# Attention and two expert layers on one core: GpSimd splits queries before values, and five pieces of operand work change their place

## What is computed

```python
# q, k, v: 4 x 8 x 576 x 64; block-causal mask, blocks of 64
scores = q @ k^T / sqrt(64); masked where block_i < block_j
x = softmax(scores) @ v                     # -> 2304 x 512
p = probs / (sum(probs) + 1e-9)
for e in range(4):
    y += p[:, e] * (relu(x @ w1[e]) @ w2[e])  # 512 -> 1024 -> 512
h = y @ w_in
ln = layer_norm(h * softmax(h)) * g_ln
out = ln @ w_out
```

## Time and profile before

| what | value |
|---|---|
| median of the runs | 1160.57 us |
| time of the profiled execution | 1159.74 us |
| its span, from first to last instruction | 1157.9 us |
| PE busy, share of the span | 1138.7 us, 98% |
| PE busy, first 185 us (attention) | 175.23 us |
| PE busy, 185 to 262 us | 73.24 us |
| PE busy, 262 to 935 us | 673.00 us |
| DVE / ACT / POOL busy, first 185 us | 165.25 / 158.05 / 163.12 us |

### The profile page before, as it was taken

One profiled execution on the slowest core, in us unless ns is written; L12 is line 12 of the kernel. 1 busy time (PEld: TensorE's weight loads), 2 busy tenths in 40 slices (PEclk: granted clock), 3 DMA queues, 4 the chain that ended last, 5 costly groups with the idle time before them and its releaser, 6 DMA issues.

```text
span 1157.9 us, 16760 instructions
## 1 busy us (share of the span) xinstructions
PE 1138.7 (98%) x6131; PEld 1020.9 (88%) x6131; DVE 633.4 (55%) x1139; ACT 428.5 (37%) x943; POOL 415.7 (36%) x403
## 2 busy tenths in 40 slices
PE   8999998989999999999999999999999999999998
PEld 7999988879999999999999999999998977888887
DVE  8999886454343424343433344353424468666765
ACT  7988885322223211122311113321112344434432
POOL 7998996654234100015300004500003463432330
PEclk9999999999999999999999999999999999999999
DMA  4766767983734222252405062503125100000001
GB/s 142 227 213 211 218 207 221 393 323 124 277 113 157 89 82 110 82 194 72 180 1 191 1 230 71 200 28 132 60 83 199 39 16 10 29 19 28 19 28 37
DMA packets 68342, 146.29 MB, mean 126 GB/s; under 512 B 6064, under 2 KB 34736, under 8 KB 68272
## 3 DMA queue, kind: packets, MB, share of 16 engines
q1 hardware_dynamic: 68272, 145.36, 36.2%
HBM read 114.60 MB, written 30.74 MB: 126 GB/s over the span
## 4 chain that ended last, share of the span: by engine, by line
PE 76%; POOL 1%; DVE 1%; DMA 1%; ACT 0%; issue 0%; SPq 0%; ACTq 0%; POOLq 0%
PE s L1723 34%; PE outp L1584 19%; PE s L1584 11%; PE ring L1584 10%; PE ring L1854 1%; DMA xr<-x_stash 1%; PE s L1797 1%; POOL x_late L761 0%; DMA x_stash<-x_tmp 0%; POOL yop_l L863 0%; DVE yop_l L1432 0%; ACT y_t L1108 0%; DVE acc L1378 0%; POOL x_tmp L785 0%; DVE ex L1504 0%
## 5 line engine op out<-in xcount | busy, mean ns | idle before, releaser
L1723 PE MATMUL s<-xr,w1s 128*128 128x384 f32 x2016 | 360.8, 337 | 4.9 <-DVE u L1414 2.5
L1723 PEld LDWEIGHTS s<-xr,w1s 128*128 128x128 f32 x2016 | 351.9, 189 | 9.7 <-DVE u L1414 2.8
L1061 ACT ACTIVATE hid_h<-u 128x384 fp32r<-128x384 f32 x96 | 50.4, 525 | 371.9 <-DVE u L1409 346.7
L720 POOL TENSOR_TENSOR work<-work 128x256 f32<-128x256 f32 x20 | 15.9, 797 | 393.8 <-DMA work<-in_moe_w 267.9
L1364 DVE SCALAR_TENSOR_TENSOR hid_l<-s,hid_h 128x384 fp32r<-128x384 f32 x48 | 26.7, 557 | 125.7 <-ACT hid_h L1057 125.7
L1723 PE MATMUL s<-w1s,yop_h 128*128 128x512 f32 x252 | 85.7, 399 | 1.9 <-POOL yop_l L863 0.7
L1322 DVE TENSOR_TENSOR u<-s,m_b 128x384 f32<-128x384 f32 x24 | 13.4, 557 | 131.9 <-PE s L1723 131.9
L1057 ACT ACTIVATE hid_h<-s 128x384 fp32r<-128x384 f32 x48 | 23.6, 491 | 155.6 <-PE s L1584 155.6
L1584 PE MATMUL s<-k_h,qb 128*128 128x288 f32 (+8 forms) x320 | 75.9, 324 | 3.3 <-ACT pr L906 1.7
L906 ACT ACTIVATE pr<-s,neg_max 128x576 f32<-128x576 f32 (+2 forms) x144 | 75.5, 537 | 3.3 <-DVE neg_max L1206 3.0
L1584 PE MATMUL outp<-w_h,hid_h 128*128 128x512 f32 x192 | 75.5, 393 | 0.0
(11 more groups left out here) (172 smaller groups left out, 2446.2 us busy)
## 6 DMA issues: line engine op xcount, KB each, us to landing
xr<-x_stash SPq DMA_DIRECT2D x77, 768.0 KB, 6.4
r_sb<-r_scratch SPq DMA_DIRECT2D x16, 576.0 KB, 4.3
x_rows<-x_n SPq DMA_DIRECT2D x32, 288.0 KB, 4.6
work<-x_rows SPq DMA_DIRECT2D x24, 384.0 KB, 6.7
x_stash<-x_tmp SPq DMA_DIRECT2D x12, 768.0 KB, 3.8
work<-in_moe_w SPq DMA_DIRECT2D x32, 256.0 KB, 3.9
stage<-in_moe_w SPq DMA_DIRECT2D x32, 256.0 KB, 5.1
x_stash<-xr SPq DMA_DIRECT2D x7, 768.0 KB, 9.8
```

What stands on the lines that cost most here:

```text
L720: pool.tensor_tensor(s1, a21, a22, ALU.add).then_inc(w1_sums, 1)
L1061: act.activation(hid[slot][0][:, :], source, ACT.Relu).then_inc(hid_high, 1)
L1723: last = pe.matmul(target, x, y, start=start and i == 0, stop=stop and i == 2, skip_group_check=True)
```

## The change

1. GpSimd's round p of the attention does `split_query(p + 2)` before `split_values(p)`. The query split no longer waits for `v_split`; at the start of a round GpSimd waits for its own last work of the round before.
2. SP issues `load_q(p + 3)` right behind `load_k(p + 2)`, before `store_r(p)`, and no longer behind `load_v(p + 1)`.
3. GpSimd's `x_low_part(0, 0, 2)` and `(0, 0, 3)` move from round 13 to round 12, before `x_join(0, 1)`. After the attention `x_join(sg + 1, 0)` moves behind `x_low_part(sg, 1, 2)` and `(sg, 1, 3)`.
4. ACT's `x_cast(0, 1, 0)` moves from the end of step 13 to its middle, `x_cast(0, 1, 3)` from the end of step 14 to `nearly_late` of it.
5. SP stores group 0's slots in the pieces 0 to 2, 3, 4, and 5 to 6, with rounds of group 1 between them, not in two pieces 0 to 2 and 3 to 6.
6. DVE's `normalise_probs` (seven small operations, L1355 to L1359) moves from unit 2 to unit 4, just before its first user.

```diff
--- before.py
+++ after.py
@@ -583,6 +583,8 @@
                     load_x(0, 1, (0,))
                 if p + 2 < PAIRS:
                     load_k(p + 2)
+                if p + 3 < PAIRS:
+                    load_q(p + 3)
                 store_r(p)
                 spread_r(p)
                 if p == 11:
@@ -593,8 +595,6 @@
                     store_x(p - 1)
                 if p + 1 < PAIRS:
                     load_v(p + 1)
-                if p + 3 < PAIRS:
-                    load_q(p + 3)
                 if p in (1, 3, 5):
                     v_ = (p + 1) // 2
                     if v_ >= 2:
@@ -622,12 +622,16 @@
             stash_round(1, 0, 1)
             sp.wait_ge(w2_ready, 4)
             load2(w2[0, :, :], 3)
-            stash_first(range(3, NP))
+            stash_first(range(3, 4))
             stash_round(1, 0, 2)
             stash_round(1, 0, 3)
             load_x(2, 0)
-            for r in range(NR):
-                stash_round(1, 1, r)
+            stash_first(range(4, 5))
+            stash_round(1, 1, 0)
+            stash_round(1, 1, 1)
+            stash_first(range(5, NP))
+            stash_round(1, 1, 2)
+            stash_round(1, 1, 3)
             load_operands(1)
             load_x(2, 1)
             for t in range(2):
@@ -687,7 +691,6 @@
                 pool.wait_ge(q_loaded[p % 2], 16 * (p // 2 + 1))
                 if p >= 2:
                     pool.wait_ge(scored, GROUPS_S * (p - 1))
-                    pool.wait_ge(v_split, p - 1)
                 else:
                     pool.wait_ge(crossed_clear, 1)
                 placed = [[heads_of(qb_l[p % 2] if z else qb_h[p % 2], 0, BLOCKS)[h * DH:(h + 1) * DH, :, h, :]
@@ -790,9 +793,21 @@
             pool.wait_ge(first_split, 3)
             split_query(1)
             for p in range(PAIRS):
-                split_values(p)
+                if p in (1, 3, 5, 7):
+                    pool.wait_ge(w1_ready, 3 * (p // 2) + 1)
+                if p in (2, 4, 6, 8):
+                    pool.wait_ge(w1_ready, 3 * (p // 2))
+                if p == 9:
+                    pool.wait_ge(v_split, 9)
+                if p in (10, 13):
+                    pool.wait_ge(x_added, 1 + p // 13)
+                if p == 11:
+                    pool.wait_ge(x_sums, 4)
+                if p == 12:
+                    pool.wait_ge(x_low, 2)
                 if p + 2 < PAIRS:
                     split_query(p + 2)
+                split_values(p)
                 if p in (0, 2, 4, 6):
                     w1_add(0, p // 2)
                     w1_low_first(0, p // 2)
@@ -808,10 +823,10 @@
                     x_low_part(0, 0, 0)
                     x_low_part(0, 0, 1)
                 if p == 12:
+                    x_low_part(0, 0, 2)
+                    x_low_part(0, 0, 3)
                     x_join(0, 1)
                 if p == 13:
-                    x_low_part(0, 0, 2)
-                    x_low_part(0, 0, 3)
                     x_add(0, 1, 0)
                     x_add(0, 1, 1)
                 if p == 14:
@@ -829,10 +844,10 @@
                     x_low_part(sg, t, 1)
                     if t == 0:
                         x_join(sg, 1)
-                    elif sg + 1 < SUPERS:
-                        x_join(sg + 1, 0)
                     x_low_part(sg, t, 2)
                     x_low_part(sg, t, 3)
+                    if t == 1 and sg + 1 < SUPERS:
+                        x_join(sg + 1, 0)
             def y_add(p):
                 t1, t2, t4 = (y_s[:, x * BLK:(x + 1) * BLK] for x in (0, 1, 3))
                 b21, b22 = y_t[:, BLK:2 * BLK], y_t[:, 3 * BLK:4 * BLK]
@@ -971,22 +986,21 @@
                     w1_cast_sums(0, p // 2)
                 if p in (10, 11):
                     x_cast(0, 0, p - 10)
-                if p == 14:
-                    x_cast(0, 1, 1)
+                if p in (13, 14):
+                    x_cast(0, 1, p - 13)
 
             def nearly_late(p):
                 if p == 11:
                     x_cast(0, 0, 2)
                 if p == 14:
                     x_cast(0, 1, 2)
+                    x_cast(0, 1, 3)
 
             def late(p):
                 if p in (0, 2, 4, 6):
                     w1_cast_plain(0, p // 2, 1)
                 if p == 11:
                     x_cast(0, 0, 3)
-                if p in (13, 14):
-                    x_cast(0, 1, 3 * (p - 13))
 
             def step(p, par, ahead=True):
                 n = p + 1
@@ -1398,9 +1412,9 @@
                         dve.wait_ge(x_low, NR * 2 * SUPERS)
                         for s in range(2):
                             dve.wait_ge(tmp_stored[s], 16 * 4 * (SUPERS - 1))
+                    if n == 1:
+                        normalise_probs()
                     accumulate(n - 1, 0, downs(m - 1, 2))
-                if m == 2:
-                    normalise_probs()
                 make_u3(m)
                 if m == 0:
                     scale_left(PAIRS - 1, 1)
```

## The result

The changed kernel takes 1155.19 us, median of 5 runs from 1152.29 to 1155.85, where the kernel before took 1160.54 beside it: a ratio of 0.9949, 95% interval 0.9935 to 0.9962. It is faster by 5.4 us, where 9.5 were forecast. The profiled execution took 1155.19 us, its span 1153.4 (before: 1157.9).

The account below looks back on a forecast made before the run. PE is busy 98% of the span, so only its waits and slow running could go: 5.3 us from stores and join plus 4.2 from the attention, 1160.57 - 9.5 = 1151.1 us; range for 8 in 10, 1148.0 to 1157.5.

Parts of the forecast that it names:

- What bounds the kernel: Whole kernel: PE is busy for 98% of the span, so only its waits and lower-clock time can be gained.
- Attention, 4.2 us: Attention, all pairs: queries first and moved x work gain 4.2 us, bounds 1 and 6.
- the lead at T8R of step 7: Attention, pairs 0 to 10: queries first put PE ahead by 0.7 us, bounds -1 and 1.5.
- Step 14: Attention, step 14: GpSimd's sums done earlier, ACT's and PE's waits go, all_right(14) comes sooner; 1.5 us.
- the last step: End of the attention: GpSimd's last low part ends earlier, PE's wait before its first `up` nearly goes; 1.3 us.
- The bounding argument that found 164.8: Attention, round 13: values end near 164.8 behind moved low parts and join, so PE is at most about 1.4 us ahead.
- The stall of unit 3, 4.19 us: Unit 3: with stores in pieces ACT's store lands earlier, so PE's wait and the slow stretch go; 4.19 us.
- The rival that the stall stays: Unit 3: the landing is late whatever stands behind, only the attention gains; 1156.4, chance 0.12.
- the one that the attention gains nothing: Attention: late values eat its gain, the gain from the stores stays; 1155.3, chance 0.05.
- normalise_probs, 0 us: Unit 4: normalise_probs before three `acc` operations is covered by DVE's spare time; 0 us, else some tenths lost.
- Unit 4, 1.07 us: Unit 4: earlier stores put the slots of m1, m6 and m2 in place before PE needs them; 1.07 us gained.
- a clock below 1 between 215 and 262 us: Units behind the attention: a granted clock below 1 at 215 to 262 us would show the forecast wrong.

Follow-up runs that it names:

- 3: Changed kernel with group 0's slots of m1, m6 and m2 stored first, the other four behind group 1's first three loads; 1157.34 us, ratio 0.9973.
- experiment 11: Kernel before with only queries split before values on GpSimd and load_q right behind load_k; 1155.83 us, ratio 0.9969.
- 1: Kernel before with only group 0's stores in pieces and x_join(2, 0) behind the low parts; 1158.04 us, ratio 0.9983.
- 6: Kernel of 1 with the x rows of group 2 loaded behind load_operands(1); 1157.51 us, ratio 0.9982.
- 9: Kernel before with stores in pieces, x_join(2, 0) behind the low parts and normalise_probs in unit 4, attention as before; 1156.95 us, ratio 0.9980.
- 4: Changed kernel with one more 768 KB copy out of xr, to a place nobody reads, behind group 0's last piece; 1156.66 us, ratio 0.9968.
- 5: Changed kernel with the load of group 2's x rows (1.57 MB) moved behind load_operands(1); 1152.04 us, ratio 0.9929.
- 7: Changed kernel with GpSimd splitting values before queries in rounds 7 and 13 alone; 1154.29 us, ratio 0.9947.
- 8: Kernel of 5 with GpSimd splitting values before queries in rounds 7 and 13; 1149.88 us, ratio 0.9918.
- 12: Kernel of 5 with GpSimd splitting values before queries in round 13 alone; 1150.36 us, ratio 0.9919.

## Why the prediction was half right

The time lies in the range (1148.0 to 1157.5) and on the faster side, but 0.7 us outside the forecast's own range, 1148 to 1154.5.

**What bounds the kernel: right.** PE's own work did not change; what moved is its waiting and its slow stretches.

**Attention, 4.2 us: right, 4.71, in part by luck.** Kernels with this attention code have m5 of unit 0 at 191.3 to 191.9, and once at 194.02 (3); those with the one before at 195.05 to 196.83. By steps: the lead at T8R of step 7 was 1.4 us (91.33 to 89.89) for 0.7 forecast, inside the bounds. At `all_right(13)` it was 2.0 for 1.4, with the values' end at 164.07 for 164.8, which did pace PE. Step 14 brought 0.8 of the 1.5 (182.68 - 171.11 = 11.57 us became 10.74), the last step 1.6 for 1.3: one term too small and one too large made the sum come out. The load of x rows no longer holds up the keys, and PE no longer waits for GpSimd before its first `up`. What the forecast did not weigh is the alternative: it took the whole block as one, and in experiment 11, without the moved low parts, the profile gains 6.2, 1.5 more. The bounding argument that found 164.8 had the term in it, 2.8 us in front of the values of pair 13.

**The stall of unit 3, 4.19 us: gone as forecast,** and ACT's store lands earlier: its cast starts at 221.04 for 230.41, 5.2 us earlier against PE, inside the 3 to 6 that the forecast named, and PE's way to m7 of unit 3 is 3.60 us shorter. The rival that the stall stays is wrong, though its time (1156.4) is near the result; so is the one that the attention gains nothing, whose 1155.3 is nearest of all.

**normalise_probs, 0 us: wrong as a term.** The seven operations took 2.7 us in unit 2 and were in time there. With the stall gone GpSimd's low parts stand beside them, the last four take 4.58 us in place of 1.41, and PE waits 1.5 us in 1 and 6. Without this move the way to m7 of unit 3 shortens by 1.94 us (1), with it by 3.61 (9): it carries 1.67 of the gain that the forecast gave to the stores alone. It was priced at its new place and not at its old one.

**Unit 4, 1.07 us: the step that failed.** The sentence was that the slots of m1, m6 and m2 are in place near 240 to 245 "and PE needs them at 246 to 248". The last stores went at 233.74, even before the forecast's 236, and the operands of m6 landed at 245.8, nearly in the range. But the need was dated too late. In the kernel before PE had m1 of unit 4 about 4.2 us behind m7 of unit 3, at 250.1; less the 4.19 of unit 3 that is 245.9, the start of the forecast's 246 to 248. With the 4.2 us of the attention, its own term, the need is at 241.7, and that is where PE stood (244.03 - 2.16 = 241.87). Supply and need were both dated with the gain behind the attention alone. And the share of 0.69 that stood for the queues was a mean over a stretch in which ACT's stall had left SP nothing to store. With the stall gone the queues are full for 50 us, and the bytes in front of the operands set their landing: with 0.79 MB more those of m6 land 1.9 us later (4), with 1.57 MB less 3.5 earlier (5). The wait comes with a slow stretch behind it, as in the kernel before; the forecast gave a clock below 1 between 215 and 262 us as a sign of being wrong, and it has shown. Between the profiles the terms miss by 4.8 us in unit 4 (1.07 forecast as gained, 3.75 lost; the 1.07 set a start of the chain, 262.41, against one of the rows, 245.86, and is 0.91 by the rows alone) and by 0.6 in unit 3, and the attention gives 0.5 back: 4.9, as 9.5 less 4.56. By the medians it is 4.1, because the profiled run of the changed kernel is its median and that of the kernel before lay 0.8 below its own.

Experiment 9 shows the consequence, at a clock of 1.00: while the operands land only 0.8 us earlier, 1.7 us gained in unit 3 does not reach the end. For the 0.5 us that 7 gains in the attention it stays open, because the clock in its profile was lower. Experiment 5 is the changed kernel without this limit, 8.2 us below before by ratio; 8 and 12 reach 9.5 and 9.4, as much as was forecast.

**Left open.** Why the attention's late steps differ by 1 to 2 us between profiles of kernels with the same code there (T8R of step 10 at 123.06 in 5 and 124.05 in 12). The kernel that the runs point to, the queries' order without part 3's first move, the stores, `normalise_probs` in unit 4 and the rows later, was not run as one. How much of the median of the changed kernel is the slow stretch and how much the waits: one execution was traced.

## What to carry to other kernels

Date every need and every supply on the same clock: when one term brings an engine forward, all that it waits for later is wanted earlier by the sum of the gains, and only what hangs on the same engine comes along. A low share of the queues behind a stall is the stall's own trace, so count the bytes from the first store to the last load and divide by the full rate before taking room for granted. And when a stall goes, the work behind it moves as well: ask what that will run beside, for a wait can come out of the gain itself.

## What the runs showed of the hardware

- The queues of one core moved 392 GB/s over 50 us, and in stretches of 2 us 433 (215 to 217 in the changed kernel) and once 437 (236 to 238 in experiment 1). The Trainium skill (DMA: Bandwidth & Descriptors, section "Specifications") gives 435 GB/s as the ceiling of the fabric and about 358 per core as the memory's limit; with one core at work the traces keep to the first within 0.5% and go beyond the second.
- Four VectorE operations on 18 columns with both inputs in SBUF took 0.84 us with GpSimd idle, 1.41 beside its sums of 1.0 to 1.5 us (kernel before), 3.58 when they ended with the first of GpSimd's two low parts, and 4.58 when they ended with the second. The Trainium skill (SBUF — State Buffer, section "Who interferes with whom") tells that such an operation contends with a GpSimd operation that reads SBUF, by a lock; the ends, 230.43 beside 230.18 in experiment 1, agree.
- The granted clock fell to 0.58 in the 3.81 us behind the waits of 2.16 and 0.55 us in unit 4, a mean over the levels of 2.4 and 1.2 GHz; in experiment 9, behind waits of 1.46 and 0.53 at about the same place, it stayed at 1.00 (245 to 255 us), and in experiment 7, behind 0.61 and 1.81, it was 0.50 from 245 to 250 us. What decides between the two no run here shows.
